# Exponential biases on ScalarE from scaled scores, reciprocals by units, low halves over two slots, a later split of the weights

## Chip, cores and metric

The kernel runs on one core of a Trainium2 chip. The metric is the device time of one execution in microseconds (us). Every matrix product is on TensorE (PE), with VectorE (DVE), ScalarE (ACT), GpSimd (POOL) and the DMA queue of SyncE (SP) around it.

## What is computed

```
scores = q @ k.T / 8                      # 4 batches x 8 heads, 576 x 576, depth 64
kth    = 32nd largest of each row
scores = where(scores >= kth, scores, -1e9); scores -= max of the row
attn   = exp(scores); attn /= sum(attn) + 1e-9
x      = attn @ v                         # heads side by side: 4 x 576 x 512
gate   = sigmoid(causal 5-tap convolution of x)
y      = (gate * (x @ w_val)) @ w_out
u      = y + real(fft2(y)); un = layernorm(u)
out    = u + relu(un @ w_ch1) @ w_ch2     # hidden width 2048
```

## The kernel before

**Tiles and slots.** Two heads form a pair, and a pair has 9 tiles of 128 rows of scores: tiles 0 to 7 alternate between the heads, tile 8 has the last 64 rows of both. There are 16 pairs and so 144 tiles, 36 for a batch. A unit is what one attention step takes: tiles (0,1), (2,3), (4,5), (6,7) and (8) of a pair, 80 in all. One loop over slots `s` is written out on every engine, and each engine does for slot `s`, in the order of its own code, what falls due. For tile `t`: slot `t` is the scores (PE, L505) and their copy to SBUF (ACT, L737, `copy_scores`); the selection of the 32 largest (DVE, `select`, MAX8 and MATCH_REPLACE8, for a pair of tiles at a time) begins at slot `t+1`; slot `t+5` has the exponential (ACT, `exponent`: Prelu L745, Exp L751); slot `t+6` the transposes (PE, L519), their copy `pT` (ACT, L759) and the reciprocal of the row sums (`reciprocal`, on POOL for the first batch, on DVE after it, L908); slot `t+7`, at the end of a unit, the attention (`attend`, PE L535 and L539), whose product is copied (ACT, L768) and scaled (POOL, L1057). Nothing but these queues and their semaphores sets the order.

**Two stages.** Slots 0 to 42 have the first batch's attention with side work: both weight matrices `w_ch1`, `w_ch2` are split into a rounded high half (ACT, L777) and a low half (POOL, L1062) in 32 parts, one a slot from slot `SPLIT_AT`; ACT waits there for the part's load, and the load of part `i+3` waits for the low half of part `i`. From slot 43 on `plan[s]` has the dense steps of the batch before beside the attention of the next (val, zed, seq, proj, trn, ch0, ch1; on DVE among others `gv` L969 and `u` L937, on ACT `un` L808 and `hid_hi` L818, on POOL `rstd`, `un_lo`, `hid_lo` L1116). After slot 150 there is only the last batch's dense work.

**Biases.** The exponential of the kept scores needs `(kth - max)/8` as a bias. POOL makes it (`biases`, L1036, slot `t+5`), behind all that POOL had in earlier slots, and ACT waits for it between Prelu and Exp.

**Reciprocals.** The row sums are in 8 columns (`NK = 8`, column `t % NK`). One reciprocal serves tiles `(t-1, t)` with `t` odd over the whole list. In pairs with an odd number, and for tile 8 of an even one, a unit ends on an even `t`, so that its attention of slot `t+7` waits (`pe.wait_ge(s_rinv, t // 2 + 1)`) for a reciprocal that also needs tile `t+1` and stands in slot `t+7` too, on DVE behind slot `t+6`'s steps.

**Low halves.** Each head's q and k are split as well: high halves on ACT, low halves `q_st` and `k_lo` both in one slot (POOL, L1014 and L1017, for even heads; POOL in the first batch and DVE later for odd ones).

Of the kernel before, what the change touches and what calls it, by code (L numbers as in the profile page):

```python
# [7 lines left out]
F32 = mybir.dt.float32  # L8
# [4 lines left out]
P = 128  # L13
# [9 lines left out]
TOPK = 32  # L23
NK = 8
# [93 lines left out]
HIGH_Q0, HIGH_K0, LOW0 = {2: 0, 5: 1}, {3: 0, 5: 1}, {3: 0, 6: 1}  # L118

SPLIT_AT, NRAW = 2, 3  # L120
# [34 lines left out]
def build(nc, qT, kT, v, w_val, conv_w, w_out, w_outT, w_ch1, w_ch2, feat, cosT, sinT, ident, out):  # L155
    with ExitStack() as ctx:
# [214 lines left out]
        with nc.Block() as block:  # L371
# [121 lines left out]
            def _(pe):  # L493
# [220 lines left out]
            def _(act):  # L714
# [18 lines left out]
                def copy_scores(t):  # L733
                    act.wait_ge(s_qk, t + 1)
                    if t >= NS:
                        act.wait_ge(s_drop, t - NS + 1)
                    act.activation(s_sb[t % NS][:, :].rearrange("p (o n) -> p o n", o=2), p_s[:, :, 0:HALF_S],  # L737
                                   ACT.Copy).then_inc(s_copy, 1)

                def exponent(t):  # L740

                    act.wait_ge(s_topk, t + 1)
                    if t >= 3:
                        act.wait_ge(s_tr, t - 2)
                    act.activation(prob[t % 3][:, 0:S], s_sb[t % NS][:, :], ACT.Prelu,  # L745
                                   bias=top[t % NK][:, TOPK - 1:TOPK], scale=-1.0, alpha=1.0 / BIG).then_inc(s_drop, 1)
                    act.wait_ge(s_bias, t + 1)
                    if t >= NK:
                        act.wait_ge(s_radd, (t - NK) // 2 + 1)
# [105 lines left out]
            def _(dve):  # L855
# [33 lines left out]
                def split_low(p):  # L889
                    dve.wait_ge(s_hi, 5 * (p + 1))  # L890
                    whole = (S // P) * P
                    q, k, high = q_st[1][p % 2], k_lo[1][p % 2], k_hi[1][p % 2]
                    q_in, k_in = raw(p, 1)
# [3 lines left out]
                    dve.tensor_tensor(k[:, :], k_in, high[:, :].bitcast(F32),  # L897
                                      ALU.subtract).then_inc(s_lo[1], 1)

                def reciprocal(t):  # L900

                    dve.wait_ge(s_exp, t + 1)
                    if t >= NK:
                        dve.wait_ge(s_pv, unit_of(t - NK) + 1)
                    if t == POOL_RECIP + 1:
                        dve.wait_ge(s_rinv, t // 2)
                    c = slice((t - 1) % NK, (t - 1) % NK + 2)
                    dve.tensor_scalar(rinv[:, c], psum_row[:, c], EPS_SUM, 2.0, ALU.add, ALU.mult).then_inc(s_radd, 1)  # L908
                    dve.wait_ge(s_radd, t // 2 + 1)
# [82 lines left out]
                split_low(0)  # L992
                for s in plan:
                    if due(s, RECIP) and (s - RECIP) % 2 and s - RECIP >= POOL_RECIP:
# [5 lines left out]
                    p, h = split_at(s, LOW0, LOW) or (0, 0)  # L1000
                    if p > POOL_PAIRS and h == 1:
                        split_low(p)
# [6 lines left out]
            def _(pool):  # L1009
                def split_low(p):  # L1010
                    pool.wait_ge(s_hi, 5 * p + 2)
                    q, k, high = q_st[0][p % 2], k_lo[0][p % 2], k_hi[0][p % 2]
                    q_in, k_in = raw(p, 0)
                    pool.tensor_tensor(q[0:D, 0:S], q_in[0:D, :], q[0:D, 0:S].bitcast(F32),  # L1014
                                       ALU.subtract).then_inc(s_lo[0], 1)
                    if p:
                        pool.tensor_tensor(k[:, :], k_in, high[:, :].bitcast(F32),  # L1017
                                           ALU.subtract).then_inc(s_lo[0], 1)

                def split_low_odd(p):  # L1020
                    pool.wait_ge(s_hi, 5 * (p + 1))
                    whole = (S // P) * P
                    q, k, high = q_st[1][p % 2], k_lo[1][p % 2], k_hi[1][p % 2]
                    q_in, k_in = raw(p, 1)
                    for to, of in ((slice(0, whole), slice(0, whole)), (slice(whole + REST, SP), slice(whole, S))):
                        pool.tensor_tensor(q[0:D, to], q_in[0:D, of], q[0:D, to].bitcast(F32),
                                           ALU.subtract).then_inc(s_lo[1], 1)
                    pool.tensor_tensor(k[:, :], k_in, high[:, :].bitcast(F32),
                                       ALU.subtract).then_inc(s_lo[1], 1)

                def biases(t):
                    pool.wait_ge(s_topk, t + 1)
                    if t >= NK:
                        pool.wait_ge(s_exp, t - NK + 1)
                    most, kth = top[t % NK][:, 0:1], top[t % NK][:, TOPK - 1:TOPK]
                    pool.tensor_scalar(bias[t % NK][:, :], kth, most, SCALE, ALU.subtract, ALU.mult).then_inc(s_bias, 1)  # L1036

                def reciprocal(t):

                    pool.wait_ge(s_exp, t + 1)  # L1040
                    if t >= NK:
                        pool.wait_ge(s_pv, unit_of(t - NK) + 1)
                    c = slice((t - 1) % NK, (t - 1) % NK + 2)
                    pool.tensor_scalar(rinv[:, c], psum_row[:, c], EPS_SUM, 2.0, ALU.add, ALU.mult).then_inc(s_radd, 1)
                    pool.wait_ge(s_radd, t // 2 + 1)
                    pool.tensor_tensor(rinv[:, c], rinv[:, c], power[:, 1:3], ALU.pow).then_inc(s_rinv, 1)
# [73 lines left out]
                split_low(0)  # L1120
                for s in plan:
                    if due(s, RECIP) and (s - RECIP) % 2 and s - RECIP < POOL_RECIP:
# [65 lines left out]
```

## Time and profile before

| | us |
|---|---|
| median of 3 runs (1098.96 to 1102.12) | 1100.66 |
| the profiled execution | 1104.79 |
| its span | 1103.0 |
| PE / DVE / ACT / POOL busy | 984.0 / 847.8 / 606.0 / 397.0 |

The span is what the profile covers; the 1.8 us around it belong to the execution's time too. Busy shares say little by themselves here, since the bound changes from stage to stage: the windows and the waits of each stage are to be read. In a row of waits "A <- B" means that A's engine sat idle until B's instruction ended; "issue" is idle time for which the profile names nobody.

### The profile page before, as it was taken

The page shows a single profiled execution, that of the slowest core. Times are in us where ns is not written, and L with a number is a line of the kernel's source. Part 1 is how long each engine was busy: PE and PEld are TensorE (multiplying, and loading weights), DVE is VectorE, ACT ScalarE, POOL GpSimd, SP SyncE. Part 2 cuts the span into 40 slices and gives each one's busy share as a digit, 9 for nine tenths or more (in the row PEclk, how much of TensorE's full clock was granted, in tenths as well). Part 3 has the DMA queues.
Part 4 walks back from the last instruction along what each step waited for, and adds up shares of the span by engine and source line. Part 5 has one row for each costly group of instructions (what it writes and reads, how often), then busy time and mean ns, then how long its engine had stood idle before and what let it go on. Part 6 is the DMA issues. An engine that isn't in the chain of part 4 may idle for free.

```text
span 1103.0 us, 19727 instructions
## 1 busy us (share of the span) xinstructions
PE 984.0 (89%) x6624; PEld 807.4 (73%) x6624; DVE 847.8 (77%) x1830; ACT 606.0 (55%) x1253; POOL 397.0 (36%) x627
## 2 busy tenths in 40 slices
PE   2776777799899999989899999999899999999997
PEld 2445565587588888866688888876688887668896
DVE  6998999988999899997997888898899972120000
ACT  3676776745467666554666656555676662022211
POOL 1676654322353333232342323232443232243221
PEclk9988878799899999999999999999999999999999
DMA  7755565211267787520578665421377775229874
GB/s 212 226 181 171 184 215 196 69 32 61 71 230 249 238 276 253 178 60 19 189 249 271 222 218 180 158 60 38 132 243 247 252 274 181 77 87 358 301 250 158
DMA packets 81187, 200.36 MB, mean 182 GB/s; under 512 B 8384, under 2 KB 26560, under 8 KB 81088
## 3 DMA queue, kind: packets, MB, share of 16 engines
q1 hardware_dynamic: 80928, 198.81, 53.5%
q8 instruction: 54, 0.88, 0.3%
q10 hardware_dynamic: 160, 0.30, 0.1%
q14 instruction: 45, 0.37, 0.1%
HBM read 177.58 MB, written 21.50 MB: 180 GB/s over the span
## 4 chain that ended last, share of the span: by engine, by line
PE 47%; issue 23%; POOL 12%; DVE 7%; ACT 5%; DMA 4%; SPq 1%; POOLq 0%; DVEq 0%; ACTq 0%
PE p_m L546 13%; PE p_m L673 9%; PE p_m L659 9%; PE p_t L535 5%; PE p_s L505 4%; PE p_t L519 3%; POOL hid_lo L1116 3%; DVE rest L875 2%; DMA w_st<-w_split 2%; POOL bias L1036 2%; DVE top L881 2%; POOL w_st L1062 2%; PE p_m L566 2%; ACT pT L759 1%; POOL q_st L1014 1%
## 5 line engine op out<-in xcount | busy, mean ns | idle before, releaser
L881 DVE MAX8 top<-rest 128x8 f32<-128x576 f32 x432 | 304.5, 746 | 0.0
L1116 POOL TENSOR_TENSOR hid_lo<-hid,hid_hi 128x256 fp32r<-128x256 f32 (+1 forms) x128 | 106.9, 836 | 305.4 <-ACT hid_hi L818 305.4
L875 DVE MATCH_REPLACE8 rest<-top,rest 128x576 f32<-128x576 f32 x288 | 211.6, 742 | 0.0
L673 PE MATMUL p_m<-w_st,hid_hi 128*128 128x512 f32 x576 | 180.1, 394 | 2.7 <-POOL hid_lo L1116 2.7
L659 PE MATMUL p_m<-un_hi,w_st 128*128 128x256 f32 (+1 forms) x1024 | 164.0, 302 | 15.0 <-ACT hid_hi L818 8.9
L659 PEld LDWEIGHTS p_m<-un_hi,w_st 128*128 128x128 f32 x1024 | 141.5, 189 | 27.5 <-issue 17.1
L737 ACT ACTIVATE s_sb<-p_s 128x576 f32<-128x576 f32 x144 | 93.3, 648 | 114.3 <-PE p_s L505 114.1
L751 ACT ACTIVATE prob<-prob,bias 128x576 f32<-128x576 f32 x144 | 111.8, 776 | 62.8 <-POOL bias L1036 50.2
L519 PE MATMUL p_t<-id_sb,prob 128*128 128x128 f32 x720 | 109.3, 285 | 29.8 <-ACT prob L751 29.8
L535 PE MATMUL p_t<-pT,v_sb 128*64 128x128 f32 (+1 forms) x1600 | 110.0, 289 | 28.4 <-ACT pT L759 17.7
L505 PE MATMUL p_s<-k_hi,q_st 128*128 128x288 f32 x320 | 110.0, 359 | 26.5 <-ACT s_sb L737 16.5
L535 PEld LDWEIGHTS p_t<-pT,v_sb 128*64 128x64 f32 x1600 | 90.2, 149 | 56.6 <-issue 33.4
L817 ACT ACTIVATE hid<-p_m 128x256 f32<-128x256 f32 (+1 forms) x128 | 51.4, 402 | 135.2 <-PE p_m L659 135.1
L519 PEld LDWEIGHTS p_t<-id_sb,prob 128*128 128x128 f32 x720 | 89.4, 146 | 36.2 <-ACT prob L751 34.9
L673 PEld LDWEIGHTS p_m<-w_st,hid_hi 128*128 128x128 f32 x576 | 100.8, 188 | 18.3 <-POOL hid_lo L1116 4.2
L673 PE MATMUL p_m<-w_st,hid_lo 128*128 128x512 f32 x288 | 113.9, 396 | 0.0
L745 ACT ACTIVATE prob<-s_sb,top 128x576 f32<-128x576 f32 x144 | 111.0, 771 | 0.0
L866 DVE MAX8 top<-s_sb 128x8 f32<-128x576 f32 x144 | 102.1, 744 | 9.7 <-ACT s_sb L737 9.7
L875 DVE MATCH_REPLACE8 rest<-top,s_sb 128x576 f32<-128x576 f32 x144 | 105.7, 741 | 0.0
L759 ACT ACTIVATE pT<-p_t 128x640 f32<-128x640 f32 x144 | 101.3, 704 | 7.0 <-PE p_t L519 7.0
L956 DVE TENSOR_TENSOR u<-p_m,u 128x512 f32<-128x512 f32 x18 | 11.5, 686 | 114.8 <-PE p_m L673 114.7
L505 PEld LDWEIGHTS p_s<-k_hi,q_st 128*128 128x128 f32 x320 | 65.0, 203 | 47.0 <-issue 31.4
(103 smaller groups left out, 1569.7 us busy)
## 6 DMA issues: line engine op xcount, KB each, us to landing
w_st<-w_split SPq DMA_DIRECT2D x256, 512.0 KB, 4.6
w_split<-w_st SPq DMA_DIRECT2D x32, 512.0 KB, 3.3
k_raw<-kT SPq DMA_DIRECT2D x62, 144.0 KB, 3.0
q_raw<-qT SPq DMA_DIRECT2D x60, 144.0 KB, 2.9
u<-w_ch SPq DMA_DIRECT2D x32, 256.0 KB, 3.7
v_sb<-v SPq DMA_DIRECT2D x16, 256.0 KB, 3.8
wslot<-w_val SPq DMA_DIRECT2D x4, 1024.0 KB, 5.4
wslot<-w_out SPq DMA_DIRECT2D x4, 1024.0 KB, 5.4
```

The costliest lines, as they stand in the source:

```text
L505: mm = pe.matmul(p_s[:, o, 0:HALF_S], q_st[h][p % 2][:, cols], k[:, o * HALF_S:o * HALF_S + HALF_S], start=n == 0, stop=n == len(parts) - 1)
L519: mm = pe.transpose(p_t[:, c * P:c * P + P], prob[t % 3][:, c * P:c * P + P], id_sb[:, :])
L535: pe.matmul(p_o[D * h:D * h + D, 0, 0:n], v_sb[p % 2][:, c, D * h:D * h + D], pT[tt % 3][:, c, c0:c0 + n], start=c == 0, stop=c == NCH - 1 ...
L546: mm = pe.matmul(bank[rows, c0:c1], a, w, start=k == 0, stop=k == len(lhs) - 1, skip_group_check=True)
L659: mm = pe.matmul(mbank(HIDDEN_BANK[g], n), w1_st[i % NB1][:, w, k, :], x[:, k, at:at + n], start=part + k == 0, stop=part + k == KC + 1)
L673: mm = pe.matmul(mbank(j), h[i % 2][:, P * j:P * j + P], w2_st[i % NB2][:, w, :], start=f == 0 and part == 0, stop=f == FC - 1 and part == 2)
L745: act.activation(prob[t % 3][:, 0:S], s_sb[t % NS][:, :], ACT.Prelu, bias=top[t % NK][:, TOPK - 1:TOPK], scale=-1.0, alpha=1.0 / BIG).then ...
L751: act.activation(prob[t % 3][:, 0:S], prob[t % 3][:, 0:S], ACT.Exp, bias=bias[t % NK][:, :], scale=-SCALE * BIG, accum_out=psum_row[:, t % ...
L759: act.activation(pT[t % 3][:, :, :].rearrange("p c n -> p (c n)"), p_t[:, 0:SP], ACT.Copy).then_inc(s_pT, 1)
L875: dve.match_replace(rest[tt % 2][:, :], top[tt % NK][:, 8 * n - 8:8 * n], src[:, :], LOWEST).then_inc(s_chain, 1)
L881: found = dve.max(top[tt % NK][:, 8 * n:8 * n + 8], rest[tt % 2][:, :])
L1116: pool.tensor_tensor(hid_lo[i % 2][:, 0:width(b, g)], hid[:, 0:width(b, g)], hid_hi[i % 2][:, 0:width(b, g)].bitcast(F32), ALU.subtract).t ...
```

## The change

ACT scales the scores by 1/8 as it copies them, so that the bias is `kth - max`, and makes the bias itself with an Identity activation of one column ahead of Prelu; POOL's `biases` is gone. `NK` becomes 9 and a reciprocal belongs to a unit and is due at the unit's last tile, slot `t+6`: 80 of them in place of 72, those of tile 8 of one column. `split_low` is cut into `low_queries` and `low_keys`, a slot apart, and loads and high halves move by one slot with them. `SPLIT_AT` goes from 2 to 5.

```
-LOAD = {7: 0, 3: 1}
-HIGH_Q, HIGH_K, LOW = {0: 0, 4: 1}, {1: 0, 5: 1}, {2: 0, 6: 1}
+LOAD = {8: 0, 4: 1}
+HIGH_Q, HIGH_K, LOW_Q, LOW_K = {0: 0, 5: 1}, {1: 0, 6: 1}, {2: 0, 6: 1}, {3: 0, 7: 1}
...
-SPLIT_AT, NRAW = 2, 3
+SPLIT_AT, NRAW = 5, 3
...
-                    pe.wait_ge(s_rinv, t // 2 + 1)
+                    pe.wait_ge(s_rinv, unit_of(t) + 1)
...
-                                   ACT.Copy).then_inc(s_copy, 1)
+                                   ACT.Copy, scale=SCALE).then_inc(s_copy, 1)
...
                     act.wait_ge(s_topk, t + 1)
+                    if t >= NK:
+                        act.wait_ge(s_exp, t - NK + 1)
+                    most, kth = top[t % NK][:, 0:1], top[t % NK][:, TOPK - 1:TOPK]
+                    act.activation(bias[t % NK][:, :], most, ACT.Identity, bias=kth, scale=-1.0).then_inc(s_bias, 1)
...
-                                   bias=bias[t % NK][:, :], scale=-SCALE * BIG,
+                                   bias=bias[t % NK][:, :], scale=-BIG,
...
                 def reciprocal(t):
+                    n = unit_end(t)
                     dve.wait_ge(s_exp, t + 1)
...
-                    if due(s, RECIP) and (s - RECIP) % 2 and s - RECIP >= POOL_RECIP:
+                    if due(s, RECIP) and unit_end(s - RECIP) is not None and s - RECIP >= POOL_RECIP:
                         reciprocal(s - RECIP)
...
-                    if due(s, EXPONENT):
-                        biases(s - EXPONENT)
```

**ACT's queue, slots 0 to 5, before.** L737 are copies of scores, L777 the high halves of the weights.

```order
8 L737 ACTIVATE s_sb<-p_s 128x576 x3
9 L777 ACTIVATE w_st<-u 128x512
10 L724 ACTIVATE q_st<-q_raw 128x576
11 L737 ACTIVATE s_sb<-p_s 128x576
12 L777 ACTIVATE w_st<-u 128x512
13 L731 ACTIVATE k_hi<-k_raw 128x576
14 L737 ACTIVATE s_sb<-p_s 128x576
15 L777 ACTIVATE w_st<-u 128x512
16 L737 ACTIVATE s_sb<-p_s 128x576
17 L745 ACTIVATE prob<-s_sb,top 128x576
18 L751 ACTIVATE prob,psum_row<-prob,bias 128x576
```

**The same slots of the changed kernel.**

```order
8 L737 ACTIVATE s_sb<-p_s 128x576 x3
9 L724 ACTIVATE q_st<-q_raw 128x576
10 L737 ACTIVATE s_sb<-p_s 128x576
11 L731 ACTIVATE k_hi<-k_raw 128x576
12 L737 ACTIVATE s_sb<-p_s 128x576 x2
13 L746 ACTIVATE bias<-top 128x1
14 L749 ACTIVATE prob<-s_sb,top 128x576
15 L755 ACTIVATE prob,psum_row<-prob,bias 128x576
16 L781 ACTIVATE w_st<-u 128x512
```

Three high halves of weights are gone from between the copies of slots 2 to 4, and the first bias and exponential of ACT stand ahead of the first of them.

**DVE's queue, slots 52 and 53, before.** The first row begins the selection of tiles 50 and 51; the `rinv` rows are the reciprocal for tiles 46 and 47, for which the attention of the unit (45, 46) waits.

```order
229 L866 MAX top<-s_sb 128x8 x2
230 L875 MATCH_REPLACE rest<-top,s_sb 128x576 x2
231 L881 MAX top<-rest 128x8 x2
232 L937 TENSOR_TENSOR u<-p_m,pm 128x257
233 L938 TENSOR_TENSOR u<-p_m,pm 128x255
234 L940 BN_STATS stats<-u 128x6
235 L942 BN_AGGR mv<-stats 128x2
236 L950 TENSOR_SCALAR un<-u,mv,rstd 128x512
...
240 L942 BN_AGGR mv<-stats 128x2
241 L908 TENSOR_SCALAR rinv<-psum_row 128x2
242 L910 RECIPROCAL rinv<-rinv 128x2
```

**The same place of the changed kernel**, where the `rinv` rows are for tiles 45 and 46.

```order
228 L916 TENSOR_SCALAR rinv<-psum_row 128x2
229 L918 RECIPROCAL rinv<-rinv 128x2
230 L870 MAX top<-s_sb 128x8 x2
231 L879 MATCH_REPLACE rest<-top,s_sb 128x576 x2
232 L885 MAX top<-rest 128x8 x2
233 L903 TENSOR_TENSOR k_lo<-k_raw,k_hi 128x576
234 L945 TENSOR_TENSOR u<-p_m,pm 128x257
```

The reciprocal has moved from behind a part of a selection and two tiles' worth of `u` to ahead of all of them, and a low half of keys has come behind the selection.

**POOL's queue, slots 65 and 66, before** (low halves of pair 8's even head between the steps of ch1).

```order
275 L1116 TENSOR_TENSOR hid_lo<-hid,hid_hi 128x256
276 L1014 TENSOR_TENSOR q_st<-q_raw,q_st 64x576
277 L1017 TENSOR_TENSOR k_lo<-k_raw,k_hi 128x576
278 L1036 TENSOR_SCALAR bias<-top 128x1
279 L1116 TENSOR_TENSOR hid_lo<-hid,hid_hi 128x256
280 L1057 TENSOR_TENSOR x_new<-or_sb 128x128
```

**And changed.**

```order
180 L1116 TENSOR_TENSOR hid_lo<-hid,hid_hi 128x256 x2
181 L1028 TENSOR_TENSOR q_st<-q_raw,q_st 64x576
182 L1116 TENSOR_TENSOR hid_lo<-hid,hid_hi 128x256
183 L1057 TENSOR_TENSOR x_new<-or_sb 128x128
184 L1033 TENSOR_TENSOR k_lo<-k_raw,k_hi 128x576
185 L1116 TENSOR_TENSOR hid_lo<-hid,hid_hi 128x256 x2
```

Between the low queries and the next `hid_lo` neither `k_lo` nor `bias` stands any more. PE's queue is the same row for row.

## Rows read from the trace of the kernel before

**Rows 1.** Windows: us; busy (count) of PE, PEld, DVE, ACT, POOL; clock; DMA; GB/s.
```profile
22.00:110.00 88.00, 61.87 (x354) 43.19 (x356) 80.65 (x168) 60.30 (x116) 57.74 (x82) 0.89 0.58 185
110.00:225.00 115.00, 84.30 (x606) 69.54 (x603) 113.53 (x238) 84.54 (x162) 55.46 (x87) 0.80 0.51 168
225.00:925.00 700.00, 666.21 (x4797) 555.51 (x4795) 617.01 (x1335) 421.51 (x885) 233.36 (x385) 0.99 0.53 178
```
**Rows 2.** Waits of 22 to 110 us: total, times, longest.
```profile
ACT w_st L777 <- DMA u<-w_ch: 12.6, 2, 7.7
ACT prob L751 <- POOL bias L1036: 7.7, 8, 2.3
DVE top L866 <- ACT s_sb L737: 7.4, 6, 3.3
```
**Rows 3.** Timeline of ACT, 22 to 44 us: start, duration, row, idle before.
```profile
22.85 0.63 ACT L777 ACTIVATE w_st<-u 128x512 fp32r<-128x512 f32 x1 [7.72 <-DMA u<-w_ch]
...
35.82 0.63 ACT L777 ACTIVATE w_st<-u 128x512 fp32r<-128x512 f32 x1 [4.86 <-DMA u<-w_ch]
...
39.58 0.78 ACT L751 ACTIVATE prob<-prob,bias 128x576 f32<-128x576 f32 x1
...
43.34 0.78 ACT L751 ACTIVATE prob<-prob,bias 128x576 f32<-128x576 f32 x1
```
**Rows 4.** Timeline of DVE: last maxima of tiles 0, 1 and of 2, 3.
```profile
20.71 1.40 DVE L881 MAX8 top<-rest 128x8 f32<-128x576 f32 x2
...
24.63 0.76 DVE L866 MAX8 top<-s_sb 128x8 f32<-128x576 f32 x1 [1.85 <-ACT s_sb L737]
...
32.30 1.41 DVE L881 MAX8 top<-rest 128x8 f32<-128x576 f32 x2
```
**Rows 5.** Groups of ACT by shape: count, busy, mean ns, idle before.
```profile
L745 ACT ACTIVATE prob<-s_sb,top 128x576 f32<-128x576 f32 x144 | 111.0, 771 | 0.0
...
L731 ACT ACTIVATE k_hi<-k_raw 128x576 fp32r<-128x576 f32 x31 | 21.1, 679 | 2.4 <-DMA k_raw<-kT 2.4
...
L727 ACT ACTIVATE q_st<-q_raw 128x64 fp32r<-128x64 f32 x15 | 3.7, 248 | 0.0
```
**Rows 6.** Waits of PE, 22 to 225 us.
```profile
PE p_t L535 <- issue: 3.7, 2, 1.9
```
**Rows 7.** Waits of DVE, 225 to 310 us.
```profile
DVE u L937 <- PE p_m L546: 6.5, 2, 3.7
DVE gv L969 <- PE p_m L546: 5.2, 3, 2.2
```
**Rows 8.** Waits of PE, 225 to 925 us.
```profile
PE p_t L535 <- issue: 7.0, 2, 3.5
PE p_m L659 <- ACT hid_hi L818: 6.9, 12, 1.5
PE p_m L598 <- DVE gv L969: 5.4, 2, 4.0
```
**Rows 9.** Timelines of PE's weight loads and DVE about 292 us.
```profile
292.50 1.18 PEld L535 LDWEIGHTS p_t<-pT,v_sb 128*64 128x64 f32 x12 [3.66 <-issue]
...
292.26 0.17 DVE L910 RECIPROCAL rinv<-rinv 128x2 f32<-128x2 f32 x1
```
**Rows 10.** Timelines about 376 us.
```profile
376.51 0.77 ACT L751 ACTIVATE prob<-prob,bias 128x576 f32<-128x576 f32 x1 [2.52 <-POOL bias L1036]
...
378.99 0.30 PEld L673 LDWEIGHTS p_m<-w_st,hid_hi 128*128 128x128 f32 x2 [2.43 <-POOL hid_lo L1116]
```
**Rows 11.** Timelines about 526 us.
```profile
526.46 0.78 ACT L751 ACTIVATE prob<-prob,bias 128x576 f32<-128x576 f32 x1 [2.85 <-POOL bias L1036]
...
528.41 0.42 PEld L644 LDWEIGHTS p_m<-id_sb,un 128*128 128x128 f32 x4 [3.49 <-issue]
```
**Rows 12.** Timeline of PE: the 20 matmuls of a unit, early and late.
```profile
117.61 2.40 PE L535 MATMUL p_t<-pT,v_sb 128*64 128x128 f32 x20 [0.88 <-ACT pT L759]
...
410.75 1.31 PE L535 MATMUL p_t<-pT,v_sb 128*64 128x128 f32 x20
```

More of the change, by code:

```diff
@@ L887, in select, with low_queries @@
                                 done[tt] = count[0]
-                def split_low(p):
-                    dve.wait_ge(s_hi, 5 * (p + 1))
+                def low_queries(p):
+                    dve.wait_ge(s_hi, 5 * p + 4)
                     whole = (S // P) * P
-                    q, k, high = q_st[1][p % 2], k_lo[1][p % 2], k_hi[1][p % 2]
-                    q_in, k_in = raw(p, 1)
+                    q, q_in = q_st[1][p % 2], raw(p, 1)[0]
                     for to, of in ((slice(0, whole), slice(0, whole)), (slice(whole + REST, SP), slice(whole, S))):
@@ L999, in _ @@
                         select(s - SELECT - 1, 1)
-                    p, h = split_at(s, LOW0, LOW) or (0, 0)
+                    p, h = split_at(s, LOW_Q0, LOW_Q) or (0, 0)
                     if p > POOL_PAIRS and h == 1:
-                        split_low(p)
+                        low_queries(p)
+                    p, h = split_at(s, LOW_K0, LOW_K) or (0, 0)
+                    if p > POOL_PAIRS and h == 1:
+                        low_keys(p)
                     for b, c, taps in conv_due(s):
@@ L1020, in split_low_odd, with low_queries @@
-                def split_low_odd(p):
-                    pool.wait_ge(s_hi, 5 * (p + 1))
+                def low_queries(p, h):
+                    pool.wait_ge(s_hi, 5 * p + (4 if h else 1 if p else 2))
                     whole = (S // P) * P
-                    q, k, high = q_st[1][p % 2], k_lo[1][p % 2], k_hi[1][p % 2]
-                    q_in, k_in = raw(p, 1)
-                    for to, of in ((slice(0, whole), slice(0, whole)), (slice(whole + REST, SP), slice(whole, S))):
+                    q, q_in = q_st[h][p % 2], raw(p, h)[0]
+                    parts = ((slice(0, whole), slice(0, whole)), (slice(whole + REST, SP), slice(whole, S)))
+                    for to, of in parts if h else ((slice(0, S), slice(0, S)),):
@@ L1026, in split_low_odd @@
                         pool.tensor_tensor(q[0:D, to], q_in[0:D, of], q[0:D, to].bitcast(F32),
[L1027 to L1036, printed above, removed]
+                                           ALU.subtract).then_inc(s_lo[h], 1)
@@ L1038, in reciprocal, with low_keys @@
+                def low_keys(p, h):
+                    pool.wait_ge(s_hi, 5 * p + (5 if h else 2))
+                    pool.tensor_tensor(k_lo[h][p % 2][:, :], raw(p, h)[1], k_hi[h][p % 2][:, :].bitcast(F32),
+                                       ALU.subtract).then_inc(s_lo[h], 1)
                 def reciprocal(t):
+                    n = unit_end(t)
                     pool.wait_ge(s_exp, t + 1)
-                    if t >= NK:
-                        pool.wait_ge(s_pv, unit_of(t - NK) + 1)
@@ L1119, in _ @@
                 pool.wait_ge(s_zero, FILLS)
-                split_low(0)
+                low_queries(0, 0)
                 for s in plan:
-                    if due(s, RECIP) and (s - RECIP) % 2 and s - RECIP < POOL_RECIP:
+                    if due(s, RECIP) and unit_end(s - RECIP) is not None and s - RECIP < POOL_RECIP:
                         reciprocal(s - RECIP)
-                    if due(s, EXPONENT):
-                        biases(s - EXPONENT)
                     if part_due(s, 1) is not None:
@@ L1135, in _ @@
                         step(*x)
-                    p, h = split_at(s, LOW0, LOW) or (0, 0)
-                    if p and h == 0:
-                        split_low(p)
-                    elif p and p <= POOL_PAIRS:
-                        split_low_odd(p)
+                    p, h = split_at(s, LOW_Q0, LOW_Q) or (0, 0)
+                    if p and (h == 0 or p <= POOL_PAIRS):
+                        low_queries(p, h)
+                    p, h = split_at(s, LOW_K0, LOW_K) or (0, 0)
+                    if p and (h == 0 or p <= POOL_PAIRS):
+                        low_keys(p, h)
         numbers = sorted(x.num for x in sems)
```

46 lines of the change are left out of this document (22 added, 24 removed).

## The prediction, made before the changed kernel ran

> **What bounds the kernel now.** I read the windows by stage first, then the waits of each stage, then single rows of the timeline for the long waits.
>
> The windows [rows 1] show three kinds of time. From 22 to 110 us PE is busy 62 of 88 us and DVE 80.7; from 110 to 225 PE 84 of 115 and DVE 113.5. So the first batch is paced by the selection on DVE, or by something that keeps exactly up with it. From 225 to 925 us PE is busy 666 of 700 us and DVE 617: there PE is the bound, with 34 us of idle time, and DVE has 83 us. Behind 925 only the last batch's dense work is left, which the change does not touch.
>
> In the first stage two loops run side by side. One is DVE's: it waits only for copies of scores, 7.4 us up to 110 us [rows 2], and for nothing from there. The other is the exchange between PE and ACT: copy, transposes, `pT`, attention, exponential. It does not wait for DVE: Prelu, which needs the finished selection, has no idle time before it in all 144 cases [rows 5]. But it is late. The first two tiles' selection ends at 22.1 us [rows 4]; the second tile's exponential starts at 39.58, and the third's at 43.34 [rows 3]. What held ACT are two waits for parts of the weights, 7.72 us in slot 2 and 4.86 in slot 5 [rows 3] (12.6 together [rows 2]), and later the bias, 7.7 us in eight places [rows 2]. This lateness reaches slot 43, where PE's dense work begins; so what the exchange gains before 225 us shifts the PE-bound stage as a whole, as long as DVE can follow.
>
> **The change, part by part.**
>
> *Later split of the weights.* Slots 2 to 4 lose their three splits, as the order of ACT's queue shows. The copy for tile 3 no longer stands behind a load, so DVE's 1.85 us before it go [rows 4]; the other copies for which DVE waited come from the late exchange, so that I count all 7.4 us of [rows 2] as DVE's gain. For the exchange, tile 1's exponential can follow tile 0's at about 25 us, but tile 2's must then wait for the second pair, whose selection ends at 33.7, now 31.9. With Prelu's 0.9 and a bias of 0.2 it starts at about 33.0 in place of 43.34: 10.3 us ahead. That is the first term. The three splits come back in slots 34 to 36, where the exchange runs without slack: 3 x 0.63 = 1.9 us [rows 3], taken in full (nothing, if ACT happens to be waiting for PE there).
>
> *Bias on ACT.* Removed in the first stage: the 7.7 us [rows 2], of which 0.6 were at the first tile, already counted: 7.1 us. Added: 144 activations of one column. The nearest row has 64 columns and takes 248 ns; from 576 to 64 columns 679 fall to 248, so 0.84 ns a column, and one column takes about 195. A per-row operand adds the 92 ns between 771 and 679 [rows 5]. That is 0.29 us each; successive activations overlap, and I take 0.2 of ACT's time, with ends of nothing (ACT was waiting) and 0.29. In the PE-ACT exchange about every second one lies between `pT` and an exponential for which PE waits, the other behind it while PE does the attention. For 34 tiles that is 17 x 0.2 = 3.4 us (0 to 10).
>
> *Reciprocals by units.* PE waited 3.7 us in two places of the first stage for something unnamed before a unit [rows 6]; `pT` was ready about half-way, so 2 us are the reciprocal's. In the second stage there are two such waits, 7.0 us [rows 8]. The one at 292.50 ends 0.07 us after DVE's reciprocal [rows 9], which stood behind a part of a selection and two `u` steps; the order now has it ahead of them, and it needs no tile behind the unit's own. `pT` takes 0.5 us of each: 6.0 us. The eight reciprocals more are hidden in DVE's 83 us [rows 1].
>
> *Low halves over two slots, and POOL without biases.* At 376 us ACT waited 2.52 us for a bias queued behind `k_lo`, and PE 2.43 for `hid_lo` behind both [rows 10]; both causes leave the place between. At 526 us ACT waited 2.85 us for a bias that stood behind other work of POOL, and PE then 3.49 for what ACT had still to copy [rows 11]; I count 2.8. The first I do not count in full, since it lies in the stretch ahead of a `zed` step at which PE waits for DVE's `gv`, 4.0 us [rows 8]; what PE gains there it would wait for again. One of the two: 2.8 us.
>
> *Cost in the second stage.* PE waits for `hid_hi` in 12 places [rows 8]; 0.2 us more in each is 2.4 us.
>
> *Can DVE follow?* By slot 43 the exchange gains 10.3 + 7.1 + 2.0 - 3.4 - 1.9 = 14.1 us. DVE gains 7.4 itself and has 6.5 + 5.2 us of waits for PE up to 310 us [rows 7], 19.1 in all. So PE keeps its 14.1, with 5 us to spare before DVE takes over.
>
> *Sum.* 14.1 + 6.0 + 2.8 - 2.4 = 20.5 us off the profiled execution's 1104.8: 1084.3. That execution is 4.1 us above the median of the runs, so that the median should go from 1100.7 to about 1080.
>
> *A rule against a row.* In [rows 12] a unit's 20 matmuls take 2.40 us after a wait of 0.88 for `pT`, and 1.31 in the second stage; the granted clock is 0.80 to 0.89 before 225 us and 0.99 behind [rows 1], so early units run at the lower of the two levels. The sum keeps the clock as it was. The Trainium skill, page "TensorE: Matmul & The Clock Gate", section "HAM oscillation — how this bites in real kernels", says that idle stretches of PE throw its clock back to half. By that rule a first stage in which PE waits less would also run at a higher clock, and one in which it waits for selections in longer pieces at a lower one; the third rival gives the price of each.
>
> *A price that only a page has.* No Identity stands in this trace. The Trainium skill, page "ScalarE: Activation LUTs", section "Table sets: the hidden batching unit", says that cheap functions, identity among them, are in every set; by it no table is loaded for the bias.
>
> **The rivals.**
>
> 1. *DVE takes over.* The exchange gains its 14 us, but DVE, which gains only 7.4, holds PE back from slot 43 on: its `gv` and `u` steps stand behind selections. For it: DVE is 98.7% busy from 110 to 225 us, and the `gv` waits of PE are DVE's already [rows 1, 8]. Against it: DVE's 11.7 us of waits up to 310 [rows 7]. Then 7.4 + about half of the later 6.4 = 10.6 us: 1090.
>
> 2. *Nothing comes through*: the loads wait later in place of earlier, and the exchange, which ran as fast as DVE from 110 us on, is no faster. For it: the load of part 3 still follows the low half of part 0. Against: between slots 5 and 8 stands a selection that ends 10 us after the first [rows 4], more than the 4.86 us of the load's wait. 1098 to 1103.
>
> 3. *The clock.* If the first stage's units ran at the full level, 18 units of 1.1 us would be another 19.6 us, of which DVE's spare 5 let 5 through, and some more gaps close behind: 1070. If it fell through the stretch from 22 to 110 us as well, 8 units of 1.1 us cost 9: 1089.
>
> 4. *Slower: the bias lies on the path.* Every bias is an instruction of ACT between the end of a selection and the exponential for which PE's transposes wait. If ACT, not PE, set the pace in both stages, 144 x 0.29 = 42 us would come and 21 go: 1120; it decides against the change once more than half of the biases, each at 0.29, are on the path. Against it: ACT is busy 421 of 700 us in the second stage [rows 1].
>
> **How the numbers follow.** Forecast as above, with its neighbours (1074 to 1086): 0.5. Rival 1 and the low clock (1086 to 1095): 0.23. Faster still, the full clock: 0.1. Rival 2: 0.09. Rival 4: 0.08. Faster by over 0.3% (3.3 us, about what a measurement of this kernel can tell) are the first three and a part of rival 2: 0.86; within: 0.07; slower: 0.07. The range leaves out rivals 2 and 4 and the far end of the fast side: 1069 to 1095.
>
> **What would show it.** Right: ACT's first bias and exponential follow the selection at 22 us within 2 us; the waits for weight loads are under 3 us; the wait for copies on DVE falls below 2; slot 43's first val matmul is some 14 us earlier; PE has no unnamed wait over 1 us before a unit; `bias` takes 0.25 to 0.3 us, 144 times. Wrong: Prelu has idle time ahead of it and the val step is less than 8 us earlier (rival 1 would show `gv` or `u` of DVE as PE's releaser), or PE's waits for `prob` grow in the second stage (rival 4).

## The result, and the profile after

The changed kernel takes 1095.56 us (median of 13 runs, 1091.76 to 1096.98); before, on the same chip, 1100.22 (13 runs, 1098.22 to 1105.06). The ratio is 0.995, with an interval of 0.9935 to 0.9964: about 5 us faster (4 to 7 by the interval), where 20.5 were forecast. The profiled execution took 1096.7 us with a span of 1094.8.

The windows by stage, as in [rows 1] (us; busy time and count of PE, PEld, DVE, ACT, POOL; granted clock; DMA share; GB/s), of the changed kernel:

```profile
22.00:110.00 88.00, 68.77 (x408) 49.55 (x407) 88.00 (x184) 68.13 (x141) 54.05 (x72) 0.85 0.60 184
110.00:225.00 115.00, 86.97 (x631) 71.88 (x631) 114.25 (x244) 87.93 (x186) 49.28 (x66) 0.87 0.51 170
225.00:925.00 700.00, 665.27 (x4764) 553.02 (x4763) 618.74 (x1336) 434.62 (x977) 190.46 (x278) 0.99 0.53 179
```

In the first stage DVE is now busy without a gap up to 110 us and but for 0.8 us behind it, and PE does 7 us more work up to 110 us. From 225 to 925 us PE is busy no more than before: 665 us against 666. What was to be gained there is absent.

ACT's timeline (start, duration, instruction, idle before it) answers to [rows 3]:

```profile
21.13 0.29 ACT L746 ACTIVATE bias<-top 128x1 f32<-128x1 f32 x1
...
22.18 0.78 ACT L755 ACTIVATE prob<-prob,bias 128x576 f32<-128x576 f32 x1
...
23.17 0.63 ACT L781 ACTIVATE w_st<-u 128x512 fp32r<-128x512 f32 x1
...
32.65 0.30 ACT L746 ACTIVATE bias<-top 128x1 f32<-128x1 f32 x1
32.83 0.78 ACT L749 ACTIVATE prob<-s_sb,top 128x576 f32<-128x576 f32 x1
33.70 0.78 ACT L755 ACTIVATE prob<-prob,bias 128x576 f32<-128x576 f32 x1
```

The waits for weight loads are gone, and the third tile's exponential starts at 33.70 us, against 43.34 before (forecast 33.0). The group of the bias by shape (count, busy, mean ns, idle before), to be set beside [rows 5]:

```profile
L746 ACT ACTIVATE bias<-top 128x1 f32<-128x1 f32 x144 | 41.8, 290 | 0.0
```

The weight load of the first val matmul starts at 210.6 us, against 225.3: 14.7 us earlier, forecast 14.1. So the profile of the first stage looks as forecast; the second does not. PE's waits from 225 to 925 us (total, times, longest), to be set beside [rows 8]:

```profile
PE p_m L659 <- issue: 10.1, 3, 4.0
PE p_m L598 <- DVE gv L977: 5.9, 2, 4.6
PE p_m L659 <- ACT hid_hi L822: 5.8, 9, 1.5
PE p_m L659 <- DMA w_st<-w_split: 5.0, 3, 2.2
```

The two unnamed waits of L535 for the reciprocal, 7.0 us, are gone. In their place stand three unnamed waits of L659, 10.1 us, at the first ch0 step of each batch. The one of the first batch, in the timeline of PE's weight loads and of DVE:

```profile
284.87 0.36 PEld L519 LDWEIGHTS p_t<-id_sb,prob 128*128 128x128 f32 x3
288.43 0.72 PEld L659 LDWEIGHTS p_m<-un_hi,w_st 128*128 128x128 f32 x3 [3.20 <-issue]
```

```profile
283.26 0.15 DVE L916 TENSOR_SCALAR rinv<-psum_row 128x2 f32<-128x2 f32 x1
283.44 0.17 DVE L918 RECIPROCAL rinv<-rinv 128x2 f32<-128x2 f32 x1
283.53 1.42 DVE L870 MAX8 top<-s_sb 128x8 f32<-128x576 f32 x2
...
286.31 1.41 DVE L885 MAX8 top<-rest 128x8 f32<-128x576 f32 x2
287.63 0.40 DVE L945 TENSOR_TENSOR u<-p_m,pm 64x257 f32<-64x257 f32 x1
287.96 0.41 DVE L946 TENSOR_TENSOR u<-p_m,pm 64x255 f32<-64x255 f32 x1
```

In `hidden`, step `f == 0` of ch0 waits for all `u` rows of its batch (`m_u`). The last of them, proj 4's, ends at 288.37 us, and PE starts 0.06 us behind it. DVE's order puts the reciprocal and then 4.1 us of selection ahead of it. The reciprocal came in time; what stood in DVE's queue behind it did not.

The wait also costs clock. Windows of the changed kernel around it:

```profile
280.00:288.00 8.00, 5.47 (x23) 2.50 (x21) 7.96 (x19) 7.10 (x15) 3.32 (x7) 0.97 0.47 166
288.00:294.00 6.00, 5.54 (x36) 5.07 (x36) 5.93 (x15) 0.69 (x3) 1.49 (x3) 0.50 0.40 140
```

For 6 us behind the wait PE runs at the lower level, 1.2 GHz, which is up to another 3 us: a wait of 3.2 us is worth 5 to 6 (5.5 by the leads below). In the kernel before, the same low clock lay behind the reciprocal's wait of [rows 9]:

```profile
292.00:298.00 6.00, 5.47 (x31) 4.22 (x32) 5.97 (x16) 2.22 (x5) 2.78 (x5) 0.50 0.03 12
```

### The profile page after: what moved, and what is told of

The parts are those of the page before. It is cut to its first block, busy times and chain, and to the rows that moved or that the text cites. A ratio compares the mean times of both kernels' runs of the same rounds, so it can differ in the third digit from the quotient of the medians.

```text
span 1094.8 us, 19607 instructions
## 1 busy us (share of the span) xinstructions
PE 988.5 (90%) x6624; PEld 810.1 (74%) x6624; DVE 851.7 (78%) x1842; ACT 633.3 (58%) x1397; POOL 345.3 (32%) x487
## 4 chain that ended last, share of the span: by engine, by line
PE 67%; DVE 20%; issue 6%; ACT 4%; DMA 2%; POOL 1%; SPq 0%; DVEq 0%; ACTq 0%; POOLq 0%
PE p_m L659 17%; PE p_m L673 16%; PE p_m L546 14%; DVE rest L879 9%; DVE top L885 7%; PE p_t L535 6%; PE p_s L505 5%; PE p_t L519 4%; DVE top L870 2%; DMA w_st<-w_split 1%; PE p_t L539 1%; PE p_m L598 1%; ACT pT L763 1%; ACT prob L749 1%; DVE gv L977 1%
## 5 line engine op out<-in xcount | busy, mean ns | idle before, releaser
L1116 POOL TENSOR_TENSOR hid_lo<-hid,hid_hi 128x256 fp32r<-128x256 f32 (+1 forms) x128 | 103.9, 812 | 331.6 <-ACT hid_hi L822 331.6
L659 PE MATMUL p_m<-un_hi,w_st 128*128 128x256 f32 (+1 forms) x1024 | 167.7, 307 | 23.9 <-issue 11.0
L673 PE MATMUL p_m<-w_st,hid_hi 128*128 128x512 f32 x576 | 182.3, 397 | 0.7 <-POOL hid_lo L1116 0.7
L659 PEld LDWEIGHTS p_m<-un_hi,w_st 128*128 128x128 f32 x1024 | 144.4, 192 | 36.8 <-issue 26.4
L737 ACT ACTIVATE s_sb<-p_s 128x576 f32<-128x576 f32 x144 | 93.2, 647 | 105.1 <-PE p_s L505 104.7
L535 PE MATMUL p_t<-pT,v_sb 128*64 128x128 f32 (+1 forms) x1600 | 108.8, 287 | 19.4 <-ACT pT L763 19.4
L535 PEld LDWEIGHTS p_t<-pT,v_sb 128*64 128x64 f32 x1600 | 89.1, 148 | 47.4 <-ACT pT L763 25.1
L505 PE MATMUL p_s<-k_lo,q_st 128*128 128x288 f32 x320 | 94.5, 310 | 0.0
```

Source lines behind the costliest of these rows:

```text
L505: mm = pe.matmul(p_s[:, o, 0:HALF_S], q_st[h][p % 2][:, cols], k[:, o * HALF_S:o * HALF_S + HALF_S], start=n == 0, stop=n == len(parts) - 1)
L535: pe.matmul(p_o[D * h:D * h + D, 0, 0:n], v_sb[p % 2][:, c, D * h:D * h + D], pT[tt % 3][:, c, c0:c0 + n], start=c == 0, stop=c == NCH - 1 ...
L659: mm = pe.matmul(mbank(HIDDEN_BANK[g], n), w1_st[i % NB1][:, w, k, :], x[:, k, at:at + n], start=part + k == 0, stop=part + k == KC + 1)
L673: mm = pe.matmul(mbank(j), h[i % 2][:, P * j:P * j + P], w2_st[i % NB2][:, w, :], start=f == 0 and part == 0, stop=f == FC - 1 and part == 2)
```

## The experiments

Medians are set against the kernel before on the same chip. Besides, I set the start of each weight load of PE in one trace against the start of the same weight load in another; "lead" below is that difference, worked out from two timelines. All the kernels here have the same weight loads in the same order, so that each has its counterpart. Kernels that ran on different chips are compared by these ratios.

**1. The kernel before and the changed kernel, profiled a second time** (no edit).

> The kernel before once more, for a second profile. Theory A (the profiled execution of before was typical up to slot 43; what the change gains there, 14.6 us, is given back later): its first val matmul comes at 225 to 227 us again, and the span differs from 1103.0 only by drift in the dense stage. Theory B (that execution was 4 us late by chance in the first stage, where the exchange between PE and ACT has no slack): the first val matmul comes at 220 to 223 us and the span is 1096 to 1100.

> The changed kernel once more, for a second profile. Theory A: first val matmul at 211 to 213 us, as in its first profile (211.7), and the 3.2 us wait of PE for the first ch0 step of batches 0 and 2 is there again. Theory B says the same of this kernel, with a scatter of 1 to 2 us, since its first stage waits for DVE's selections more evenly. In both the matmuls' own rate may differ by about 1% between executions.

They took 1100.3 and 1095.5 us. The first val matmul stood at 222.0 and 207.7 us. The first is within what the second theory gave (220 to 223); the other is 2.9 us earlier than in the first trace of that kernel, more than either theory allowed. So the profile of before that the prediction read was 3.3 us late in its first stage, the first profile of the changed kernel was late by nearly as much, and single traces move by some 3 us there. From here on the second trace of before (span 1098.5) is the reference of every lead. Against it the changed kernel leads by 11.4 and 14.3 us at the first val matmul, and by 4.1 and 5.5 at 936 us. The second stage gives back 7 to 9 us; the forecast had it gain 6.4.

**2. The later split alone, and all but the later split.**

```
p_split: the kernel before,  SPLIT_AT = 2 -> 5
a_split2: the changed kernel, SPLIT_AT = 5 -> 2
```

> The kernel before with the split of the weights three slots later, nothing else. Theory A: ACT's waits of 7.7 and 4.9 us for loads go, so that slot 43 comes 6 to 9 us earlier; the second stage is unchanged; ratio 0.992 to 0.996. Rival: the lateness is not ACT's waits but the bias and the exchange itself, and only 2 us of DVE's waits for copies go: ratio 0.998 to 1.0.

> The changed kernel with the split of the weights back in slot 2. Theory A: loses 6 to 9 us at slot 43, and so nearly all that the change gained: ratio to before 0.998 to 1.003. Rival (bias on ACT gives the gain of the first stage): ratio 0.995 to 0.997, as the whole change.

The split alone: ratio 0.9968 (0.995 to 0.9986), 1097.45 us. That lies between what the theory and its rival expected. Its lead is 8.9 us from 50 to 190 us, against 10.3 forecast for the start and 8.4 once the splits have come back, but falls to 3.6 by the first val matmul. Against the first trace of before it is 8.1 us at 190 and 6.9 at the first val matmul, so that most of the fall is the reference's own: the second trace of before ran from 190 to 222 us at a granted clock of 0.95, the first at 0.79.

All but the split: 1110.11 us, ratio 1.0066 (1.0041 to 1.0091), slower than before, and slower than the theory (0.998 to 1.003) or its rival expected. In this trace ACT waits in slot 36 for a load of queries and keys, and PE for ACT. The timelines of SP's issues, of ACT and of PE's weight loads:

```profile
174.51 0.44 SPq L477 DMA_DIRECT2D wslot<-w_val  x1
177.28 0.80 SPq L422 DMA_DIRECT2D w_st<-w_split  x2
...
179.13 0.47 SPq L387 DMA_DIRECT2D q_raw<-qT  x1
179.64 0.60 SPq L388 DMA_DIRECT2D k_raw<-kT  x1
```

```profile
189.74 0.68 ACT L724 ACTIVATE q_st<-q_raw 128x576 fp32r<-128x576 f32 x1 [5.16 <-DMA k_raw<-kT]
```

```profile
191.61 1.58 PEld L535 LDWEIGHTS p_t<-pT,v_sb 128*64 128x64 f32 x16 [6.44 <-ACT pT L763]
```

`LOAD = {8: 0, ...}` issues these loads in slot 35 and no longer in 34, and so behind the load of `w_val` and the first loads of split weights, which with `SPLIT_AT` 2 stand in slot 34. With 5 these come in slot 37, behind the queries and keys, and the changed kernel's trace has no such wait. So the two parts depend on each other; I had summed them. The profiled executions of this kernel and the changed one lie 11.2 us apart, their medians 14.6. In the traces 6.6 us of it are there at 195 us, ahead of this wait, from the later start, and 4.8 come at the wait.

**3. The u step ahead of the selection**: the test of the cause. DVE does proj 4's `u` step behind the reciprocal and ahead of the selection in its slot.

```
                    if due(s, RECIP) and unit_end(s - RECIP) is not None and s - RECIP >= POOL_RECIP:
                        reciprocal(s - RECIP)
+                   early = [x for x in plan[s] if x == ("proj", x[1], NR - 1)]
+                   for x in early:
+                       step(*x)
                    if due(s, SELECT) and (s - SELECT) % 2:
...
                    for x in plan[s]:
-                       step(*x)
+                       if x not in early:
+                           step(*x)
```

> The changed kernel with one change of order on DVE: in the slot of each batch's last proj step its u step stands ahead of the part of the selection in that slot, not behind it. Theory (DVE's order took the second stage's gain): in the changed kernel PE waited 3.2, 4.25 and 3.25 us ahead of the first ch0 step of the three batches, with DVE's u step of 64 rows ending last. These waits fall below 1 us each, about 7 to 9 us go in the trace between 281 and 780 us, and the median comes to 1087 to 1090 against 1095.6. Rival (something else, DVE's whole work or POOL's un_lo, holds PE there, or the time returns as a wait a little behind): the waits go but the next selection is late for ACT's exponential or for gv, and the median stays within 1094 to 1097.

1083.3 us (6 runs, 1080.04 to 1085.7), ratio 0.9835 (0.9806 to 0.9863). The theory's waits are gone, and more came back than it expected. Timeline of PE's weight loads, then of DVE:

```profile
283.44 0.60 PEld L519 LDWEIGHTS p_t<-id_sb,prob 128*128 128x128 f32 x5
284.01 1.01 PEld L659 LDWEIGHTS p_m<-un_hi,w_st 128*128 128x128 f32 x8
```

```profile
282.26 0.17 DVE L918 RECIPROCAL rinv<-rinv 128x2 f32<-128x2 f32 x1
283.10 0.42 DVE L945 TENSOR_TENSOR u<-p_m,pm 64x257 f32<-64x257 f32 x1 [0.68 <-PE p_m L546]
283.44 0.40 DVE L946 TENSOR_TENSOR u<-p_m,pm 64x255 f32<-64x255 f32 x1
```

PE no longer stops there. The window from 225 to 925 us has 4 us more of PE's work in it:

```profile
225.00:925.00 700.00, 669.34 (x4799) 554.28 (x4798) 619.64 (x1341) 432.53 (x975) 196.87 (x284) 0.99 0.53 180
```

**4. The reciprocals by pairs of tiles, all else as changed.**

```
-NK = 9
+NK = 8
-                    pe.wait_ge(s_rinv, unit_of(t) + 1)
+                    pe.wait_ge(s_rinv, t // 2 + 1)
(reciprocal on DVE and POOL, its place and ACT's wait as before)
```

> The changed kernel with reciprocals by pairs of tiles and eight columns as before, all else as changed. Theory (in the second stage the reciprocal's 3.7 us wait was only the last of several that end within a microsecond or two, and its removal uncovered the wait for DVE's u step): PE waits for rinv again at about 292 and 778 us, the wait of 3.2 us just ahead is partly there too, and the median is 1095 to 1099, at most 3 us above the changed kernel. Prediction's own term (6.0 us in the second stage, 2.0 in the first): 1102 to 1104.

1092.88 us, ratio 0.9924 (0.9896 to 0.9952). Against the changed kernel's 0.995 this is no loss; if anything a gain, with intervals that overlap. The reciprocal's wait is back:

```profile
277.16 2.03 PEld L535 LDWEIGHTS p_t<-pT,v_sb 128*64 128x64 f32 x20 [3.68 <-issue]
```

and the first ch0 step, 13 us later, follows with no idle time ahead of it. In the first batch PE waits once in either kernel. The expectation's theory holds in its mechanism, though it expected 1095 to 1099 us, a loss of up to 3. In the second batch the wait ahead of the first ch0 step is there all the same, 3.21 us; experiment 6 has its cause.

**5. The u step moved, with reciprocals by pairs**: in the changed kernel with edit 4, and in the kernel before.

> The changed kernel with the last u step ahead of the selection, and the reciprocals by pairs as before. Theory (the reciprocals by unit are worth their term of 6.0 us of the second stage once DVE's u step no longer stands behind the wait that they uncover): PE waits 3.7 us for rinv again at about 277 and 755 us and the median is 4 to 7 us above the 1083.3 of the same kernel with reciprocals by unit. Rival (the kernel with the u step moved would not need them: the 12 us come from the u step alone): within 2 us of 1083.

> The kernel before with one change of order on DVE: the last u step of each batch ahead of the selection's part in its slot. Theory (this order pays only where the reciprocals are made by unit, because with pairs the reciprocal for the next unit then stands behind the selection and PE waits for it a second time): PE waits 3.7 us for rinv both at about 290 and at about 306 us, and again in the third batch, and the median is 1099 to 1104 against 1100.9. Rival (the u step's order is worth its 8 to 12 us whatever the reciprocals do): 1089 to 1093.

With the changed kernel's other parts 1100.84 us, ratio 0.9993 (0.9971 to 1.0015): 17 us worse than experiment 3, where I had expected 4 to 7. In the traces 9.5 us of it lie between 281 and 311 us, and 9.6 between 765 and 790: at both places PE has two waits more than in experiment 3. In the kernel before 1111.14 us, ratio 1.0083 (1.0057 to 1.0109), 7 us beyond the upper end of what I expected. There PE's weight loads wait twice within 20 us:

```profile
287.74 2.03 PEld L535 LDWEIGHTS p_t<-pT,v_sb 128*64 128x64 f32 x20 [3.68 <-issue]
...
306.24 0.88 PEld L535 LDWEIGHTS p_t<-pT,v_sb 128*64 128x64 f32 x16 [3.77 <-issue]
```

and in the third batch again, 3.72 and 3.76 us. DVE's timeline beside the second wait, of the kernel with the changed kernel's other parts:

```profile
287.81 0.42 DVE L943 TENSOR_TENSOR u<-p_m,pm 64x257 f32<-64x257 f32 x1 [5.72 <-PE p_m L546]
...
292.17 1.41 DVE L885 MAX8 top<-rest 128x8 f32<-128x576 f32 x2
...
293.69 0.17 DVE L916 RECIPROCAL rinv<-rinv 128x2 f32<-128x2 f32 x1
```

DVE, first in its queue the `u` step, waits 5.72 us for proj 4, which PE reaches late because of the reciprocal; then the selection comes, and only behind it the next reciprocal, for which PE waits (its unit starts at 293.92). The four kernels make a square, by ratio:

```
                         u step behind selection   u step ahead
reciprocals by pairs     0.9924                    0.9993
reciprocals by unit      0.995                     0.9835
```

The u step alone costs 8 us, the reciprocals by unit alone 3, which the intervals don't tell from nothing, and both together gain 10. That settles where the 6.0 us of the first and third batch went.

**6. The biases.** First on ACT without the other parts, then back on POOL in the changed kernel, then on POOL beside the moved u step.

```
q_bias5:    the kernel before + SPLIT_AT = 5 + scaled scores, biases on ACT
l_poolbias: the changed kernel, on POOL in the exponential's slot:
+   pool.tensor_scalar(bias[t % NK][:, :], kth, most, 1.0, ALU.subtract, ALU.mult).then_inc(s_bias, 1)
u_pool:     l_poolbias + the u step ahead of the selection
```

> The kernel before with the later split of the weights and with scaled scores and the biases on ACT; reciprocals by pairs and low halves in one slot as before. The later split alone was at 1097.4. Theory (the bias on ACT gains in the first stage what POOL's biases held, and loses 0.1 us a slot where PE is the bound): against the later split alone the offset grows by 4 to 7 us up to 225 us and falls by 4 to 5 us from there to 936 us; median 1095 to 1098. Rival (the bias on ACT costs nothing in the second stage): the offset holds and the median is 1090 to 1093.

> The changed kernel with the biases made on POOL again (one subtraction of the two scaled scores), all else as changed. Theory (each bias on ACT costs PE about 0.1 us a slot where PE is the bound, by pT and hid that come later): the slow loss of 1.4 us from 572 to 733 us and of 2 us from 815 to 936 us is gone, so about 4 to 5 us come back in the second stage; in the first stage the waits for POOL's biases return, up to 7 us, so the median is 1094 to 1099. Rival (the slow loss comes of the reciprocals by unit or the low halves over two slots): the slow loss stays and the median is 1098 to 1103.

> The changed kernel with the last u step ahead of the selection, and the biases made on POOL. Theory (biases on ACT cost more in the second stage than they save in the first; on POOL with everything else changed the kernel stood 4 us better): 1077 to 1081, the first stage 3 us later than with ACT's biases, the second 6 us shorter. Rival (what POOL's biases gained there was a shorter wait for the u step, 1.8 instead of 3.2 us, which is already gone here): 1083 to 1086.

They took 1098.78 us (ratio 0.9964, 0.994 to 0.9987), 1091.79 (0.9901, 0.987 to 0.9933) and 1088.2 (0.987, 0.9843 to 0.9897), each outside both of its expected ranges: the first and the last above, the second below.

On top of the later split alone, 0.9968, the bias on ACT brings nothing: the first val matmul stands at 218.7 us against 218.4. That holds for low halves in one slot. With low halves over two slots the first val matmul is 3.0 and 5.9 us earlier with ACT's biases (the two traces of the changed kernel) and 5.4 earlier with the u step moved: about the forecast's 7.1 - 3.4.

The trace of the first, `q_bias5`, shows one thing more. The kernel before has an idle stretch of 3.5 us at 528 us, behind a bias of POOL [rows 11]. Here it is gone, and in its place PE waits for the first ch0 step of the second batch, again right behind DVE's `u` step, though its reciprocals are by pairs (timelines of PE's weight loads, then of DVE):

```profile
527.17 1.05 PEld L659 LDWEIGHTS p_m<-un_hi,w_st 128*128 128x128 f32 x6 [4.13 <-issue]
```

```profile
524.89 1.41 DVE L885 MAX8 top<-rest 128x8 f32<-128x576 f32 x2
526.34 0.43 DVE L943 TENSOR_TENSOR u<-p_m,pm 64x257 f32<-64x257 f32 x1
526.69 0.42 DVE L944 TENSOR_TENSOR u<-p_m,pm 64x255 f32<-64x255 f32 x1
```

So in the first and third batch the reciprocals by unit uncovered the wait for `u`, and in the second the biases on ACT did.

With everything changed POOL's biases are 5 us better; with the u step moved they are 4 us worse, though there the intervals overlap. The trace of the second suggests why the sign turns; it is of the slowest of that kernel's six runs, and at 936 us it leads the two traces of the changed kernel by 1.9 and 0.5 us only. POOL's biases make ACT wait in the first stage,

```profile
ACT prob L752 <- POOL bias L1024: 8.7, 10, 2.3
```

PE comes 3 us later to the val steps (213.6 us), and at the first ch0 step it then waits less for the same DVE queue (the row names POOL's `un_lo`, but DVE's last `u` ends at 291.36 us):

```profile
291.43 0.65 PEld L659 LDWEIGHTS p_m<-un_hi,w_st 128*128 128x128 f32 x5 [1.80 <-POOL un_lo L1111]
```

A wait of 1.80 us instead of 3.20, and 2.0 us of lead lost between 300 and 311 us instead of 5.5 and 4.4. So most of the lead that ACT's biases gave is spent at the next place that DVE sets; the rest of the 5 us between the medians is not shown.

**7. The low halves in one slot, with the loads as before**, beside the moved u step.

```
-LOAD = {8: 0, 4: 1}
+LOAD = {7: 0, 3: 1}
(HIGH and LOW tables as before, in both batches)
```

> The changed kernel with the last u step ahead of the selection, and the low halves in one slot with the loads as before. Theory (the term of 2.8 us for the low halves over two slots holds, at 376 or 526 us): 1085 to 1088, with a wait of over 2 us for hid_lo or prob near 376 or 526 us again. Rival (with the biases off POOL nothing stands behind its low halves any more, so their place is worth nothing): 1082 to 1085.

1087.25 us, but from 1082.17 to 1094.88 (6 runs), ratio 0.9875 (0.9838 to 0.9913), against 0.9835 with low halves over two slots: by its time within both the theory's and the rival's reach. The theory's sign did not come: no wait of over 2 us stands near 376 or 526 us, and the lead rises there as with two slots (3.6 and 2.6 us). A cleaner pair for the first stage is already there: q_bias5 and l_oldrinv differ in the low halves and loads alone. The first val matmul stands at 218.7 against 209.9 us: 8.8 us, for a part to which I had given none there. At 936 us 4.6 of them are left, as the ratios have it, 0.9964 against 0.9924, with intervals that just overlap. Windows from 110 to 225 us of the two, one slot first, two slots behind:

```profile
110.00:225.00 115.00, 85.59 (x583) 70.87 (x582) 108.91 (x229) 85.17 (x177) 47.45 (x60) 0.80 0.51 166
```

```profile
110.00:225.00 115.00, 86.68 (x636) 71.55 (x636) 114.93 (x246) 89.09 (x189) 49.30 (x64) 0.88 0.51 170
```

With one slot PE is busy as long and does 53 matmuls less, at a clock of 0.80 against 0.88, and DVE has gaps of 6 us in all. Whether the clock fell because of the later work or the work came later because of the clock these runs don't tell.

## Why the prediction was wrong

The leads over the second trace of before (us), at times of that trace, show the stages ("val" is the first val matmul):

```
                            val   281   300   311   523   526   545   765   776   790   816   936
changed                    11.4  11.4  17.3  11.8  10.8  13.4   8.7   8.3  11.4   8.6   6.4   4.1
changed, second trace      14.3  12.4  18.3  14.0  16.4  18.9  13.0  11.8  14.9   9.5   7.7   5.5
reciprocals by pairs       12.1  12.1  12.1  12.2  14.6  17.2  13.4  13.3  12.0  12.2   7.5   6.3
u step ahead               14.6  12.6  18.5  18.5  18.1  20.6  19.8  18.6  21.7  21.8  17.6  15.4
u step ahead, by pairs     13.7  12.6  13.8   9.1  12.7  15.2  13.9  12.5  10.8   6.1   2.2   0.9
POOL's biases               8.4   8.4  12.9  10.9  11.2  11.9  11.3  11.3  13.7  11.0   7.1   6.0
later split                 3.6   3.6   4.8   4.8   5.0   5.0   4.3   3.5   2.1   2.1   2.3   2.3
later split, ACT's biases   3.4   3.4   4.9   5.0   6.7   9.2   4.6   3.1   3.0   3.1   2.9   1.7
```

*The step that failed: what PE would meet behind the waits that go, above all behind "Reciprocals by units ... 6.0 us".* The terms of the second stage came, and were larger than forecast. Where the reciprocal's waits of [rows 9] stood, the changed kernel gains 5.9 us (281 to 300) and 3.1 (765 to 776): 9.0 against 6.0, since the low clock behind the first wait goes too. But I said of that wait only that its own producer would be early, and not what PE would meet next: some 10 us on stands a step that needs DVE's last `u`, behind a reciprocal and a part of a selection in DVE's queue. I gave that wait nothing. It takes back 5.5 us from 300 to 311, 4.8 from 526 to 545 and 2.8 from 776 to 790, 13.0 in all, and 15.8 in the second trace (4.4, 6.0 and 5.4). With the u step ahead nothing goes at the first and third place and 0.8 us at the second. I had written that a rival would be DVE taking over, priced it as a shift of the whole stage, and argued against it from the 11.7 us that DVE waits for PE up to 310 us. That is a sum over a stretch; at the place DVE is full, 7.96 of 8 us from 280, and it took over in three places only.

*Low halves over two slots, and POOL without biases, 2.8 in the second stage.* I counted one of two waits; both went, and the lead rises at each: 3.6 us from 373 to 380, and 2.6 at 523 to 526. The first goes as well with low halves in one slot and ACT's biases (`q_bias5`, 3.1; experiment 7, 3.6) as with two slots and POOL's biases (`l_poolbias`, 3.6), so that either edit is enough. The second is the biases' alone: 2.6 us in each of the eight traces with biases on ACT, 0.7 with POOL's, nothing with the split alone. It was given back at once, to the `u` step of the second batch.

*Costs of the second stage, 2.4 for `hid_hi`.* PE's waits for it went from 6.9 to 5.8 us, so it is not there. A slow loss is instead, about 2 us from 573 to 733 and 2.2 from 816 to 936, in both traces of the changed kernel. From 816 to 936 it splits cleanly: nothing with the later split alone, 1.1 to 1.3 us with only the biases on ACT, 1.0 with only the reciprocals by unit, 2.2 to 2.5 with both. So the eight reciprocals more were not free, as I had them. From 573 to 733 the biases on ACT alone cost 0.8 us; the rest is not told apart. A cost that I did not have at all: from 790 to 816 us each of the eight traces with the loads a slot later loses 1.8 to 4.7 us, with PE waiting for a load of split weights (2.40 us at 800.81 in the changed kernel), and the four others with the loads as before at most 0.3. How the loads bring it about was not followed.

*Sum of the first stage, 14.1: right in size, wrong in its parts.* The four pairs of traces give 11.4 to 17.6 us at the first val matmul, 14.5 in the mean. Start and splits, 10.3 - 1.9: 8.9 up to 190 us, and 3.6 or 6.9 at the first val matmul by the trace of before. Bias, 7.1 - 3.4: nothing with low halves in one slot, 3.0 to 5.9 with two. Low halves, counted as nothing in this stage: 8.8 with ACT's biases. Reciprocals by unit, 2.0: no more than traces differ by. These parts lean on each other and don't add up one by one, so that the sum came out owes something to chance.

*Bias activation*: 0.29 us forecast, 0.290 measured, 0.18 to 0.20 of ACT's time each. No table load came with it: either trace has one, at 2.0 us.

*Rivals.* 1 was the right one in kind, local instead of general. 2 and 4 did not come. 3: the clock moved both ways, from 0.89 to 0.85 up to 110 us and from 0.80 (0.85 in the second trace of before) to 0.87 from there to 225, and neither of its prices came. The range ended where rival 1 in its general form ended, 0.6 us below the median.

With the u step moved as well the median is 1083.3 us, below both kernels and near the forecast's 1080, but by other parts: it leads by 14.6 us at the first val matmul, where 14.1 were forecast, and gains less than 1 us from there to 936, where 6.4 were.

## What to carry to other kernels

A wait that is removed is worth only the time until the next thing for which the same engine waits. Before a number is written down, follow the waiting engine forward for 10 to 15 us and ask for each of its waits what stands ahead of the releaser in that engine's queue; an engine's idle time over a stage says nothing about it. Edits that move waits along one chain have no price of their own: time them in a square, as one edit that alone cost 8 us and one that alone gave nothing gained 10 together here. And read a term where it acts: the lead's step at 523 us was 2.6 us in eight traces, while the whole leads of two traces of one kernel lay 5.5 us apart there.

## What the runs showed of the hardware

- Behind a wait of PE of 3.2 to 4.3 us the granted clock can stand at its lower level: 0.50 from 288 to 294 us of the changed kernel, 0.57 from 523 to 527. Behind the wait of 3.25 us in the third batch it did not fall, but in the second trace, behind 3.26 us at the same place, it did (windows behind the second wait, behind the third, and behind the third in the second trace):

```profile
523.00:527.00 4.00, 3.85 (x20) 3.88 (x21) 3.87 (x11) 0.80 (x3) 1.32 (x4) 0.57 1.00 359
774.00:780.00 6.00, 6.00 (x56) 5.44 (x56) 5.96 (x14) 2.27 (x6) 2.60 (x5) 1.00 0.32 98
```

```profile
770.00:776.00 6.00, 5.76 (x37) 5.23 (x38) 5.93 (x15) 0.71 (x3) 1.49 (x3) 0.50 0.39 125
```

  So the same wait of the same kernel cost 2.8 us of lead in one execution and 5.4 in another. The Trainium skill, page "TensorE: Matmul & The Clock Gate", section "HAM oscillation — how this bites in real kernels", says that idle stretches of PE throw its clock back to half; the first two places agree with it, and the third in the second trace but not in the first.
- An activation of one column with a per-row operand takes 0.29 us, against 0.248 for one of 64 columns without one [rows 5]; the next instruction of ACT starts 0.18 to 0.20 us behind its start.
- Two traces of one kernel differ by up to 5.9 us at the same instruction (before) and 5.5 (changed) while their whole times differ by 0.4% and 0.1%. So the whole lead in one pair of traces tells no term of some 5 us; a step of the lead at one place can, where it repeats from trace to trace.
